# Attention and two feed-forward layers on one core: the first layer in chunks of 256, 256, 512 and 512 tokens, attention in units of a head pair and 128 queries

## What is computed

```python
keep = is_sink | in_window                  # 4 sink tokens, window of 128 positions
scores = np.where(keep, scale * q @ k.T, -1e9)
a = exp(scores - max); a = a / (sum(a) + 1e-9)
x = (a @ v) as [1536, 512]
h = x @ w_in;  g = where(h >= 1, h, where(h <= -1, 0, (h + 1)**2 / 4));  y = g @ w_out
h = y @ w_in2; g = where(h > 0, h, exp(min(h, 0)) - 1);                  out = g @ w_out2
```

## Time and profile before

| | |
|---|---|
| median of 3 runs | 654.17 us (654.07 to 654.3) |
| the profiled execution | 657.06 us, span from first to last instruction 655.4 us |
| busy | PE 635.3 us (97%), PEld 562.6, DVE 378.3 (58%), ACT 350.0 (53%), POOL 74.3 |
| instructions | PE 4164, DVE 994, ACT 830, POOL 147 |
| moved by DMA | 42.48 MB, mean 65 GB/s |

### The profile page before, as it was taken

The page is one execution under the profiler, slowest core; times in us unless marked ns, Lnnn a source line. Parts: engine busy times, 40 slices in busy tenths (PEclk is TensorE's granted clock), DMA queues, the critical chain, the costliest instruction groups (busy, mean ns, idle before and its releaser), DMA issues.

```text
span 655.4 us, 12200 instructions
## 1 busy us (share of the span) xinstructions
PE 635.3 (97%) x4164; PEld 562.6 (86%) x4164; DVE 378.3 (58%) x994; ACT 350.0 (53%) x830; POOL 74.3 (11%) x147
## 2 busy tenths in 40 slices
PE   5789999999999999999999999999999999999997
PEld 3688889999999999999999988888888888888886
DVE  6799968886886788588757863322332222322221
ACT  5687756665665666566656563333443333533333
POOL 4111221320322122123000000000000000000000
PEclk9799999999999999999999999999999999999999
DMA  7674212320322222122044600000100000100001
GB/s 277 188 221 143 69 39 85 91 77 24 100 65 63 62 66 86 38 77 86 25 161 161 188 7 0 1 0 1 49 16 0 0 0 0 64 0 0 0 0 64
DMA packets 15275, 42.48 MB, mean 65 GB/s; under 512 B 2852, under 2 KB 4536, under 8 KB 15248
## 3 DMA queue, kind: packets, MB, share of 16 engines
q0 software_dynamic: 7040, 20.57, 10.7%
q1 hardware_dynamic: 8208, 21.56, 9.8%
HBM read 38.98 MB, written 3.15 MB: 64 GB/s over the span
## 4 chain that ended last, share of the span: by engine, by line
PE 88%; DVE 9%; ACT 1%; issue 1%; DMA 0%; ACTq 0%; SPq 0%; DVEq 0%
PE h_ps L507 13%; PE h_ps L509 13%; PE h_ps L508 13%; PE y_ps L522 10%; PE y_ps L524 9%; PE y_ps L523 9%; PE s_ps L524 3%; PE s_ps L523 3%; PE s_ps L522 3%; PE o_ps L490 3%; PE t_ps L470 2%; DVE wout_lo L840 1%; PE s_ps L461 1%; PE s_ps L460 1%; DVE win_lo L840 1%
## 5 line engine op out<-in xcount | busy, mean ns | idle before, releaser
L507 PE MATMUL h_ps<-x_hi,win_hi 128*128 128x256 f32 (+1 forms) x576 | 186.9, 324 | 0.4
L509 PE MATMUL h_ps<-x_hi,win_lo 128*128 128x256 f32 (+1 forms) x576 | 185.2, 321 | 0.0
L508 PE MATMUL h_ps<-x_lo,win_hi 128*128 128x256 f32 (+1 forms) x576 | 184.2, 320 | 0.0
L522 PE MATMUL y_ps<-g_hi,wout_hi 128*128 128x256 f32 (+1 forms) x480 | 147.1, 306 | 1.7 <-DVE g_lo L853 1.6
L524 PE MATMUL y_ps<-g_hi,wout_lo 128*128 128x256 f32 (+1 forms) x480 | 146.4, 305 | 0.0
L523 PE MATMUL y_ps<-g_lo,wout_hi 128*128 128x256 f32 (+1 forms) x480 | 145.9, 304 | 0.0
L870 DVE SCALAR_TENSOR_TENSOR g_full<-g_full,h_ps 128x512 f32<-128x512 f32 x48 | 33.1, 690 | 156.6 <-ACT g_full L675 156.6
L507 PEld LDWEIGHTS h_ps<-x_hi,win_hi 128*128 128x128 f32 x576 | 108.7, 189 | 10.6 <-DVE g_full L866 1.0
L508 PEld LDWEIGHTS h_ps<-x_lo,win_hi 128*128 128x128 f32 x576 | 109.2, 190 | 9.4
L509 PEld LDWEIGHTS h_ps<-x_hi,win_lo 128*128 128x128 f32 x576 | 108.9, 189 | 8.3
L662 ACT CAST g_hi<-g_full 128x256 fp32r<-128x256 f32 (+1 forms) x144 | 68.5, 476 | 68.6 <-DVE g_full L870 34.2
(11 more groups left out here) (109 smaller groups left out, 819.2 us busy)
## 6 DMA issues: line engine op xcount, KB each, us to landing
ks<-in_k POOLq DMA_DIRECT2D x40, 260.0 KB, 3.0
raw<-in_w_in SPq DMA_DIRECT2D x11, 512.0 KB, 4.3
raw<-in_w_out SPq DMA_DIRECT2D x11, 512.0 KB, 3.5
qs<-in_q POOLq DMA_DIRECT2D x40, 128.0 KB, 2.8
vals<-in_v POOLq DMA_DIRECT2D x20, 192.0 KB, 3.1
out_y<-xy SPq DMA_DIRECT2D x12, 256.0 KB, 2.1
xy<-in_w_in SPq DMA_DIRECT2D x5, 512.0 KB, 4.9
xy<-in_w_out SPq DMA_DIRECT2D x5, 512.0 KB, 4.0
```

The lines of the kernel that those rows point to most:

```text
L507: pe.matmul(o, win_hi[:, k, f], x_hi[:, k, :], start=(k == 0), stop=False)
L508: pe.matmul(o, win_hi[:, k, f], x_lo[:, k, :], start=False, stop=False)
L509: last = pe.matmul(o, win_lo[:, k, f], x_hi[:, k, :], start=False, stop=(k == KT - 1))
L522: pe.matmul(o, wout_hi[:, t, cols], g_hi[:, t % GR, :], start=begin, stop=False, skip_group_check=True)
```

## The change

The first layer now takes chunks of 256, 256, 512 and 512 tokens (`CHUNKS0`), 64 tiles in all instead of 96. The first two are called narrow here and the other two wide. Attention is cut into 40 units, each a head pair and 128 queries (`UNITS`), where before it was 40 heads of 256 queries, so a unit has the same number of scores, exponentials and transposes as a head had. `SCORES_AT` sets their tiles: 12 of them begin in chunk 0, one in every tile of chunk 1 and one in each of the first 12 tiles of chunk 2. Scores are plain float32 products of 64 rows, one head in the upper and one in the lower half of the array's rows, with no rounding and subtraction of keys and queries ahead of them. `kept` is a copy on DVE of the sinks' probabilities. The three masks are made once and no longer copied per chunk, and the ReLU is written where the bent value goes, so that it waits for the low part of two tiles before.

The banks are shared out anew. A wide chunk needs four for y; `o_ps` serves transposes, sinks and values there, and chunk 2 has one bank for the hidden tile where before there were two. A narrow chunk has two (`h_bank` and `y_ps[3]`), takes sinks and values in `y_ps[2]`, and transposes in `o_ps`.

```diff
 CT = 256
-NC = TOK // CT
-CPB = SEQ // CT
+BLOCKS = TOK // CT
+BPB = SEQ // CT
 CT1 = 512
+CHUNKS0 = ((0, CT), (CT, CT), (2 * CT, CT1), (2 * CT + CT1, CT1))
+NC0 = len(CHUNKS0)
...
+UNITS = (BLOCKS - 1) * PAIRS * QB
+SCORES_AT = [1, 2, 3, 5, 6, 7, 9, 10] + [u + 4 for u in range(PAIRS * QB, UNITS)]
+def units_at(tile, later=0):
+    return [u for u in range(UNITS) if SCORES_AT[u] + later == tile]
+def sinks_at(tile):
+    return [u // QB for u in units_at(tile, 2) if u % QB == QB - 1]
+def pairs_at(tile):
+    return [u // QB for u in units_at(tile, 3) if u % QB == QB - 1]
...
-BESIDE = attention_plan([2, 3, 5, 6, 8, 9, 11, 12])
...
+        def h_places(layer, c):
+            if is_narrow(layer, c):
+                return [h_bank[:, 0:CT], y_ps[3][:, 0:CT]]
+            if layer == 0 and c < NC0 - 1:
+                return [h_bank[:, :]]
+            return [h_bank[:, :], s_ps[0][:, :]]
...
+        def side_bank(tile):
+            return y_ps[2] if is_narrow(0, tile // FT) else t_ps
...
-            def scores(c, h):
-                pe.wait_ge(qk_lo_ready, heads_before(c, h) + 1)
-                if not begins(c, h):
-                    pe.wait_ge(exp_done, heads_before(c, h) * QB)
+            def scores(u):
+                m, j = u // QB, u % QB
+                pe.wait_ge(qk_loaded[m % 2], (m // 2 + 1) * 16)
+                if u > 0:
+                    pe.wait_ge(exp_done, u * 2)
+                start = CT + j * SW
+                for hh in range(2):
+                    dims = slice(HD * hh, HD * (hh + 1))
+                    last = pe.matmul(s_ps[hh][:, 0:SW], qk[dims, m % 2, j * P:(j + 1) * P], qk[dims, m % 2, start:start + SW],
+                                     start=True, stop=True)
+                last.then_inc(scores_ready, 1)
+            def transposes(u):
+                j = u % QB
+                if u > 0:
+                    pe.wait_ge(probs_t_copied, u)
+                if u >= QB:
+                    pe.wait_ge(x_written, u // QB)
+                for hh in range(2):
+                    pe.wait_ge(probs_ready, u * 2 + hh + 1)
+                    for n in range(2):
+                        at_col = (hh * 2 + n) * P
+                        last = pe.transpose(t_ps[:, at_col:at_col + P], probs[:, j, hh, keys_at(hh, n)], ident[:, :])
+                last.then_inc(probs_t_ready, 1)
+            def transpose_sinks(m, tile):
+                pe.wait_ge(sinks_kept, (m + 1) * QB)
+                pe.wait_ge(probs_t_copied, (m + 1) * QB - (1 if is_narrow(0, tile // FT) else 0))
+                if m > 0:
+                    pe.wait_ge(x_written, m)
                 for j in range(QB):
-                    q, cols = q_parts[:, j * P:(j + 1) * P], slice(j * SW, (j + 1) * SW)
-                    pe.matmul(s_ps[j][:, 0:SW], q, k_hi[:, cols], start=True, stop=False)
-                    pe.matmul(s_ps[j][:, 0:SW], q, k_lo[:, cols], start=False, stop=True).then_inc(scores_ready, 1)
...
+            def beside_hidden(tile):
+                narrow = is_narrow(0, tile // FT)
+                for m in pairs_at(tile):
+                    values(m, tile)
+                for u in units_at(tile, 2):
+                    if narrow or u % QB == QB - 1:
+                        transposes(u)
+                if narrow:
+                    for m in sinks_at(tile):
+                        transpose_sinks(m, tile)
+            def beside_outward(tile):
+                narrow = is_narrow(0, tile // FT)
+                for u in units_at(tile, 2):
+                    if not narrow and u % QB == 0:
+                        transposes(u)
+                if not narrow:
+                    for m in sinks_at(tile):
+                        transpose_sinks(m, tile)
+                for u in units_at(tile):
+                    scores(u)
...
+            def exponents(u):
+                j = u % QB
+                if u >= QB:
+                    act.wait_ge(probs_t_ready, u - QB + 1)
+                    act.wait_ge(sinks_kept, u - QB + 1)
+                act.wait_ge(neg_max_ready, u + 1)
+                for hh in range(2):
+                    nc.scalar.activation(probs[:, j, hh, :], s_ps[hh][:, 0:SW], ACT.Exp, bias=tops[:, j, hh, 0:1],
+                                         accum_out=totals[:, j, hh, 0:1]).then_inc(exp_done, 1)
...
+            def write_x(m, tile):
+                act.wait_ge(attn_ready, m + 1)
                 act.sem_inc(waited_act, 1)
-                nc.scalar.copy(chunk(c)[:, p, :], o_ps[:, 0:CT]).then_inc(x_written, 1)
-            def before_layer(c, t):
...
+                    tile = c * FT + t
+                    if t > 0:
+                        part_hi(0, c, t - 1, c)
+                    for u in units_at(tile, 1):
+                        exponents(u)
+                    activate(0, c, t, c)
+                    for m in pairs_at(tile):
+                        write_x(m, tile)
+                    for u in units_at(tile, 2):
+                        copy_probs_t(u)
+                    for m in sinks_at(tile):
+                        copy_sinks(m, tile)
+                    if t == 0 and c > 0:
+                        write_y0(c - 1)
+                    for i in (SPLITS0[c](t) if SPLITS0[c] else ()):
+                        split_weights(i)
+                part_hi(0, c, FT - 1, c)
...
+                if u >= 2 * QB:
+                    dve.wait_ge(sinks_t_ready, u // QB - 1)
+                dve.wait_ge(probs_ready, (u + 1) * 2)
+                nc.vector.tensor_copy(kept[:, u // QB % 2, j, :], probs[:, j, :, :].rearrange("p h n -> p (h n)")[:, WIN:WIN + 2 * NS]).then_inc(sinks_kept, 1)
...
+                    tile = c * FT + t
+                    if t > 0:
+                        part_lo(0, c, t - 1, c)
+                    for u in units_at(tile, 1):
+                        normalise(u)
+                    activate(0, c, t, c)
+                    for m in sinks_at(tile):
+                        split_sinks(m, tile)
+                    for i in (SPLITS0[c](t) if SPLITS0[c] else ()):
+                        split_weights(i)
+                    for u in units_at(tile):
+                        maxima(u)
+                part_lo(0, c, FT - 1, c)
```

More of the change, by code:

```diff
@@ L47 @@
 RAW = 6
+RAW1 = 5
 GR = 3
@@ L208, in begins, with keys_at @@
-        def begins(c, n):
-            return isinstance(c, int) and c == 1 and n == 0
+        def keys_at(hh, n):
+            start = hh * NS + n * P
+            return slice(start, start + P)
         size = KT * GW
-        own = [raw[:, r, :] for r in range(2)]
         lent_early = [xy[:, k, TOK - size:TOK] for k in range(KT)]
-        lent_late = [raw1[:, r, :] for r in range(3)]
-        RAW1 = len(own) + len(lent_late)
+        early = [r[:, :] for r in raw0] + lent_early
         FEW = RAW - 1
@@ L224, in raw_buffer @@
         def raw_buffer(i):
-            return (own + (lent_early if i < NW else lent_late))[place[i]]
+            return early[place[i]] if i < NW else raw1[:, place[i], :]
         def raw_count(i):
@@ L232, in splits_until_free @@
         def splits_until_free(i):
-            return max([e + 1 for e in range(i) if place[e] == place[i]], default=0)
+            return max([e + 1 for e in range(i) if place[e] == place[i] and (e < NW) == (i < NW)], default=0)
         def w_parts(n):
@@ L417, in _ @@
+            build_mask(masks[:, 2, :], hidden_sinks=0)
+            pool.sem_inc(mask_ready, 1)
+            load_qk(0)
+            load_qk(1)
+            load_values(0)
+            load_values(1)
+            for m in range(2, UNITS // QB):
+                load_qk(m)
+                load_values(m)
         @block.tensor
@@ L677, in write_y @@
-            def write_y(layer, c, at_chunk):
-                if layer == 0:
-                    act.wait_ge(y_step, c * FT + FT)
-                    act.sem_inc(waited_act, 1)
-                    for n, bank in enumerate(y_ps):
-                        nc.scalar.copy(chunk(at_chunk)[:, 2 * n:2 * n + 2, :],
-                                       bank[:, :].rearrange("p (m t) -> p m t", m=2)).then_inc(y_written, 1)
+                    nc.scalar.activation(g, g, ACT.Exp, scale=-1.0).then_inc(expm_ready, 1)
@@ L712, in layer_chunk, with second_layer_chunk @@
+            def second_layer_chunk(c, splits=None):
+                for t in range(FT):
+                    if t > 0:
+                        part_hi(1, c, t - 1)
+                    activate(1, c, t)
                     for i in (splits(t) if splits else ()):
                         split_weights(i)
+                part_hi(1, c, FT - 1)
             act.wait_ge(half_set, 1)
             act.wait_ge(zeros_set, 1)
-            nc.scalar.activation(t_ps[:, 0:1], half[:, :], ACT.Exp)
+            nc.scalar.activation(o_ps[:, 0:1], half[:, :], ACT.Exp)
@@ L933 @@
     n_sink, window = int(n_sink), int(window)
-    first = [(c // CPB, (c % CPB) * CT) for c in range(NC)]
```

(1 more changed line is left out.)

626 lines of the change are left out of this document (252 added, 374 removed).

## The result

| | before | after |
|---|---|---|
| median of the runs | 654.16 us (654.07 to 654.3, 4 runs) | 679.37 us (677.4 to 683.25, 4 runs) |
| the profiled execution, its span | 657.06, 655.4 us | 683.25, 681.5 us |

The ratio is 1.038, with a 95% interval of 1.0353 to 1.0407. The kernel is 25 us slower, twice what was forecast, and outside the range. The runs of after lie 6 us apart.

A forecast was written before the change was run, and what follows sets the result against it. Chunk 0 was taken as bound by DVE, all else by TensorE; first-layer chunks 79.9 + 83.7 + 116.1 + 89.9 = 369.6 against 357.3 added 12.3 to 654.17: 666.5 us, range 660 to 672, 8 in 10 at 652 to 677.

The forecast's parts named there:

- The scores' price: TensorE, each attention unit: 0.60 us, made of 0.53 for 260 columns at full rate and the change of type.
- The sum by it: TensorE, scores with full drains at mode changes: some 0.15 us more a unit, 4 us over 28 units; not used.
- Chunk 1's loop: Chunk 1, waits between DVE, ACT and TensorE: 5.4 and 4.85 us, 10.25 per two tiles, 83.7 for the chunk.
- Waits absorbed: Rival, chance 0.17: values' copy costs nothing in chunk 1, ACT's weights are in time in chunk 0; 653.8 us.
- Faster: Rival, chance 0.15: besides, exponentials are ready when DVE comes, saving chunk 0's 7.0 us; 646.8, up to 651.
- The exposed exponentials: Chunk 0, DVE between maxima and normalise: 0.98 less 0.34 for g_lo, 0.64 x 11 = 7.0 us idle.
- The waits for ACT's weights: Chunk 0, DVE's split waits for ACT in tiles that make weights behind a copy of transposes: 4.2 us more.
- TensorE's balance: First layer, TensorE's own work: wide products take 4.2 us off for two chunks, attention adds 4.2; these cancel.
- The clock: Rival, chance 0.03: clock falls in chunk 0; for 10 us of work it costs 5, most inside DVE's wait.
- chunk 2's idle time: Chunk 2, TensorE: only the first two tiles have no outward group, 1.6 us on 114.5 of work, 116.1 in all.
- `kept` with normalise: DVE, each unit: the new copy takes 0.26 us, 1.20 with normalise.
- the smaller loads: Loads of keys, queries and values per pair have two tiles, over 9 us, to land; costed at nothing.

The follow-up runs named there:

- a1_again: The changed kernel, unchanged, profiled once more: 678.99 us.
- e4: The changed kernel with the scores of the twelve units of chunk 2 computed twice: 683.95 us (one run).
- e7: The changed kernel with one float32 product of 128 rows by 128 columns added in tiles 2 to 14 of chunk 3: 684.24 us (one run).
- e3: The changed kernel without the x_written wait ahead of narrow chunks' transposes, and with DVE's split of weights behind the maxima: 658.36 us, ratio 1.0047.
- e6: The changed kernel with two float32 products of 64 rows by 128 columns added in tiles 2 to 14 of chunk 3: 693.09 us (one run).
- e8: The changed kernel with two rounded-type products of 64 rows by 128 columns added in tiles 2 to 14 of chunk 3: 684.41 us (one run).
- e1: The changed kernel without the wait for x_written ahead of the transposes in the two narrow chunks: 665.71 us, ratio 1.0164.
- e5: The kernel of e3 with narrow chunks' scores right behind the transposes, ahead of the outward group: 656.68 us, ratio 1.0032 to the kernel before.

## Why the prediction was wrong

The forecast for the first layer was 369.6 us; in a1_again it is 83.19 + 89.25 + 119.43 + 89.24 = 381.1, so 11.5 is missing there: 3.3 in chunk 0, 5.6 in chunk 1, 3.3 in chunk 2, and 0.7 too much in chunk 3. The forecast was the time of the profiled execution less 2.9 for its distance to the median; a1_again has no such 2.9, but its start and second layer are 2.0 shorter than that execution's. 666.5 + 11.5 + 2.9 - 2.0 = 678.9, against 678.99 measured. The kinds of waits were right; four terms were too small, and the largest of them is the first.

- **The scores' price is the step that failed.** The text took 0.60 us a unit, from an early row of scores scaled by the transposes behind it. It was made of 0.53 for columns and 0.07 for the change of type; the runs show 0.43 for columns (e4), nothing for the type (e7) and 0.40 for the way into the 64-row form and back (e3, e6). That is 0.23 x 28 = 6.4 us of TensorE's work outside chunk 0, and about 4.8 us of time: in chunk 2 it shows whole, 12 x 0.23 = 2.8 of the 3.3 us by which it was longer, and in chunk 1 one unit of each two tiles stands in the loop, 8 x 0.25 = 2.0. The prediction argued from the values' entry (0.08) that a change of form is cheap; the entry of the scores is the same (0.09), but the 0.64 inside and the 0.10 behind were not in that row. The Trainium skill, "TensorEngine Tiling (Array Packing)", Key Properties, says that changing the tiling mode drains TensorE. The sum by it had 0.15 more a unit, the right direction and two thirds of the size; e6 to e8 show that the change costs 0.40 us, which agrees with the rule, but not that it is a drain.
- **Chunk 1's loop was right in kind, 0.62 us short a pair of tiles.** The order of events in the timeline is the forecast one, and e1 shows that the wait for the values' copy sets it. The tile with the values takes 5.76 us from maxima to maxima (154.86 to 160.62) against 5.4: the outward group with the scores' entry is 1.60 against 1.44 and scores to maxima 0.76 against 0.60, while the rest nearly cancels. The other takes 5.11 (149.75 to 154.86) against 4.85: maxima and exponentials with their hand-overs are 2.26 against 2.09, the activation 0.91 against 0.80. Eight times 0.62 is 5.0 of the 5.6 us missing there. *Waits absorbed* is refuted by e1: the wait cost 9.0 us in this chunk. *Faster* is refuted with it, and by the exponentials of chunk 0.
- **Chunk 0 was 3.3 us longer in a1_again, 6.5 in the profiled run.** The exposed exponentials cost 0.85 in each of 11 units, 9.3 us, not 0.64 and 7.0; the order of DVE gives back 8.3 (e1 to e3). The waits for ACT's weights were 2.3 + 1.6 = 3.9, forecast 4.2. Not in the sum at all was the wait for x_written in this chunk: TensorE idles 3.3 us ahead of the transposes, and without the wait (e1, at a clock of 0.98) the chunk took 79.17 instead of 83.19 (at 0.97). It had been priced in chunk 1 alone. That the miss stayed at 3.3 is in part luck: the rest of the sum was 2 us too long (without both waits the chunk takes 70.90 in e3, and 79.9 less the 7.0 for the exponentials is 72.9).
- **TensorE's balance.** The text lets the wide chunks take 4.2 off for two; 93.86 less 89.6 is 4.2 for each, 8.5 for both, and 2 x 4.62 = 9.2 was measured. It put the old scores at about 0.57 a head, where the trace of before has 0.47. Outside chunk 0 the scores now take 28 x 0.83 = 23.2 us of TensorE, before 32 x 0.47 = 15.0, and these 8.2 use up most of the 9.2. Neither slip enters the forecast, which goes by chunks, but they hid how little the change could gain, and so why e5, with the waits gone, is still no faster.
- **The clock** was given 0.03 and a cost hidden in DVE's wait. It fell in chunk 0 of every profile of this code. Its cost was as small as thought in the run near the median and about 3 us in the worst, so it widens the runs more than it moves the median. That it fell because TensorE idled is argued from the rows (4.53 of 6.80 us busy ahead of the fall, where the kernel before had 5.85 and no fall), and from the profiles of e3 and e5, which have none in chunk 0; no run isolates it. Their other executions had mean clocks down to 0.990, with 3 to 4 us more, and where in them the clock fell isn't on record.
- **Right:** chunk 3 at 89.24 for 89.9, chunk 2's idle time of 1.45 us for 1.6, `kept` with normalise at 1.20 (152.01 to 153.21), the smaller loads that are late nowhere in the first layer, and the direction.

## What to carry to other kernels

When an operation moves to another form of the array, price the excursion, not the columns: what the next product waits counts as well, and it is paid each time, however few columns are inside. Ahead of moving work off an engine, ask what that work covered: here the subtractions for keys and queries were about 9.3 us of DVE's time in chunk 0 (8 by 1.16), and stood with the split of weights where the exponentials were made. A wait that a bank's sharing needs in one stage should not be written into stages where the banks differ: removing it where it guarded nothing gave 13.7 of the 25 us (679.37 to 665.71, medians of two sets of runs).

## What was not expected of the hardware

- Two products of 64 rows, one in each row half, rounded type and 128 columns, put between products of 128 rows, cost 0.46 us; a float32 product of 128 rows and as many columns 0.22. Of e6's 0.63 only about a third is columns.
- Two heads' scores in the two row halves start at the same moment and take 0.43 us for 260 float32 columns each once TensorE is in that form (e4), the column rate of one product of 128 rows (e7: 0.22 for 128 columns).
- Switching between the rounded type and float32 at 128 rows costs nothing that these runs can show (e7: 0.22 for columns that take 0.21).
- The load of weights for the first product in another row form starts with that product (e8, 345.51) and not one product ahead, as it does within a form (e7, 347.41 for 347.64).
- The granted clock fell to 0.50 for 6.8 us at a time in the middle of a chunk in which TensorE was busy 74 of 86 us.
